# Top-32 threshold on folded scores in an attention + ELU-MLP + routed-experts kernel

## The chip, the cores and the metric

One Trainium2 chip, one core of it. The metric is the device time of one launch in microseconds (us), the median of several runs. Slots, tiles and lines are named as in the kernel; lines are those of the kernel before unless "after" is written.

## What is computed

The reference chains three stages; only the parts that matter here are shown. The change is in the mask of the attention and in the ELU.

```python
# attention: q, k, v are (4, 8, 576, 64), fp32
scores = scale * np.matmul(q, k.transpose(0, 1, 3, 2))
kth = np.partition(scores, -32, axis=-1)[..., -32:-31]   # 32nd largest of a row of 576
scores = np.where(scores >= kth, scores, -1e9)
attn = np.exp(scores - scores.max(-1, keepdims=True))
attn = attn / (attn.sum(-1, keepdims=True) + 1e-9)
x = np.matmul(attn, v)                                   # -> 2304 rows of 512
# dense MLP with ELU, 512 -> 2048 -> 512
h = x @ w_in
g = np.where(h > 0, h, np.exp(np.minimum(h, 0)) - 1)
x = g @ w_out
# then: each row is routed to the best of 8 experts (512 -> 1024 -> 512, ReLU) and weighted
```

## The kernel before, in words

Every engine has its program written out by hand (direct instructions, one queue for each engine, semaphores between them). The attention is cut into 144 **tiles**: 4 batches x 4 pairs of heads x 9 tiles (`PT_`). Tiles 0 to 7 of a pair are 128 query rows of one head, so two tiles (the two heads) make a **group** that shares its transposed result; tile 8 is mixed, with the last 64 rows of both heads. All engines walk the same list of **slots** s = 0, 1, ... (`END` of them). In slot s the engines work on different tiles, a software pipeline:

- TensorE (PE): the scores of the next group, 128x288 halves (`score`, L470) into two PSUM banks `sc`; `turn` (L489) transposes the five 128x128 pieces of `probs` of tile s-2 and, in the last tile of a group, a sixth piece with the reciprocals of the row sums (`rec_b`, L498); `weigh` (L501) multiplies a finished group by the values.
- ScalarE (ACT): `score_evac` (L673) copies the score halves to `scores` (five buffers); `expo` (L684) makes exp(scale*score - max) into `probs` (two buffers); `turned` (L691) copies the transposed tile.
- VectorE (DVE): `slot` (L890). The 32nd largest score of a row is found by MAX8 (the eight largest, L844) and MATCH_REPLACE8 (takes these eight out, L848): four MAX8 and three MATCH_REPLACE8 over all 576 scores. Tiles s and s-1 are interleaved, so that an instruction mostly waits for the one before the last. `mask` (L856) then multiplies the exponentials by (score >= 32nd largest) and sums the row; `total`, `reciprocal` and `normalise` finish a group.
- GpSimd (POOL): `widen` (L351) spreads the reciprocals; `split_x` (L344) and `split_w_in` (L360, eight times in slots 4, 8 to 32) split operands of the MLP into two parts.
- SyncE loads; it gates nothing here.

The MLP of batch b runs **beside** the attention of batch b+1: from slot `LAG` + 36 on, each slot also takes two of 71 positions of a schedule (`mlp_schedule`, L222): 16 "hidden" chunks (12 matmuls of 128x288 each), then "down" parts (3 or 4 matmuls in fp32), this twice, with the "rows" steps (transpose, sums, logits) in between and at the end. In each slot position 0 comes ahead of `turn`, position 1 behind it. A hidden chunk is turned into ELU by two ScalarE Relu (of -h and of h; the second frees the PSUM bank), an Exp, and on GpSimd `elu` (L389, two operations: e-1, then added to relu(h)). The MLP of the last batch runs after the last slot, alone (PE starts it at 910.26 us), with VectorE doing the last step of the ELU (L933). After it come the routing and the experts, which the change does not touch.

So what sets the order around the change is the place of each call in the slot loops of the four engines, and the waits. The lines of the order that count:

```python
# ScalarE, before (L759)                 # VectorE, before (slot, L890)
prep; score_evac(G, 0)  (even t)         eight(new,0); total; eight(old,2); reciprocal
x_high; mlp position 0                   bias(new); without(new,0); without(old,2)
turned(s-2)                              eight(new,1); eight(old,3); without(new,1)
score_evac(G, 1)  (odd t)                normalise; mask(old)      # new = s, old = s-1
expo(s); mlp position 1
```

Of the kernel before, what the change touches and what calls it, by code (L numbers as in the profile page):

```python
# [5 lines left out]
ALU = mybir.AluOpType  # L6
# [7 lines left out]
P = 128  # L14
TOP_K = 32
NEG = -3.0e38


def attention_moe_program(nc, q, k, v, w_in, w_out, emb, tau, w1, w2, out):
# [26 lines left out]
    LAG = 6  # L46
# [5 lines left out]
    with ctx:  # L52
# [13 lines left out]
        top = sbuf(ctx, "top", [P, 2, TOP_K])  # L66
# [21 lines left out]
        q_t = sbuf(first, "q_t", [P, 2, FULL * P])  # L88
# [4 lines left out]
        work = sbuf(first, "work", [P, 2, S])  # L93
# [4 lines left out]
        elu_e = sbuf(first, "elu_e", [P, HS])  # L98
# [33 lines left out]
        def bank(name):  # L132
# [15 lines left out]
        rowmax, exp_done, mask_done, rec_done = (  # L148
            sem("rowmax"), sem("exp_done"), sem("mask_done"), sem("rec_done"))
# [5 lines left out]
        elu_neg, elu_exp, elu_less = sem("elu_neg"), sem("elu_exp"), sem("elu_less")  # L155
# [53 lines left out]

        def x_at(t, b, pair, tok, n, parts=slice(0, P)):  # L210
            at = (NPAIR * b + pair) % RING * S + tok
            return t[parts, at:at + n]
# [3 lines left out]
        XT = 3  # L216
# [5 lines left out]
        def mlp_schedule():  # L222
# [13 lines left out]
            used, numbered = [0, 0], []  # L236
            for ops in positions:
                numbered.append([])
                for kind, blk, i, part, parts in ops:
                    bank_ = 0 if kind == "rows" else i % 2  # L240
                    if kind == "rows":

                        numbered[-1].append((kind, blk, i, used[1], 0, used[0]))
                        used[0] += 1
                        continue
                    numbered[-1].append((kind, blk, i, part, parts, used[bank_]))
                    if part == parts - 1:
                        used[bank_] += 1
            return numbered, used

        MLP_POSITIONS, BANK_USES = mlp_schedule()
# [8 lines left out]
        EARLY_SUMS = [op[5] + 1 for ops in MLP_POSITIONS for op in ops if op[0] == "rows"][RB - 1]  # L260
# [13 lines left out]
        def _(sp):  # L274
# [30 lines left out]
            sp.dma_start(work[0:E, 0, 0:DM], emb).then_inc(emb_in, 16)  # L305
# [36 lines left out]
        def _(pool):  # L342
# [7 lines left out]

            def widen(G):  # L351
# [37 lines left out]
            def elu(mb, m, pos):  # L389
                for kind, blk, i, *_ in mlp_at(m, pos):  # L390
                    if kind == "hidden":
                        chunk = FC * 2 * mb + (FC * blk + i)
                        e, r = elu_e[:, :], g[:, i * HS:(i + 1) * HS]
# [705 lines left out]
```

## Time and profile before

| | |
|---|---|
| median of 3 runs | 1387.83 us (1387.81 to 1389.81) |
| the profiled execution's own time | 1388.3 us |
| its span in the profile (first to last instruction) | 1386.6 us |
| busy, share of the span: PE, DVE, ACT, POOL | 88%, 67%, 39%, 18% |
| mean granted TensorE clock | 0.931 of full speed |

How to read it: the profile is one execution, so its instructions add up to the span of 1386.6 us; what lies around the span is 1.7 us. The busy shares are averages over stages that are limited by different engines, so the table of stretches and the timeline of one engine say more than they do. The "busy" time of an instruction goes from its start to its result; on all engines the next instruction may start before that, so costs are read from the distance of two starts. Of a group "idle before" is time in which its engine did nothing ahead of it.

### The profile page before, as it was taken

How to read it: one execution, taken by the hardware profiler on the slowest of the kernel's cores; microseconds unless marked ns; L12 is line 12 of the kernel's file. 1: busy time of each engine (PE TensorE's matmuls, PEld its weight loads, DVE VectorE, ACT ScalarE, POOL GpSimd, SP SyncE). 2: the span in 40 equal slices, each digit the busy share in tenths (PEclk: the TensorE clock that was granted, in tenths of full speed). 3: DMA queues.
4: the chain of work that ended last, by engine and by line, in shares of the span. 5: the costliest groups of instructions: out<-in, count | busy, mean ns of one | idle time of the engine just before them, and what ended most of it. 6: DMA issues, size and time to landing. Idle time of an engine off the chain costs nothing.

```text
span 1386.6 us, 21604 instructions
## 1 busy us (share of the span) xinstructions
PE 1213.3 (88%) x7809; PEld 937.1 (68%) x7810; DVE 932.9 (67%) x2320; ACT 543.0 (39%) x1243; POOL 247.0 (18%) x391
## 2 busy tenths in 40 slices
PE   3656666799999999999999999999984999999996
PEld 2444444586787786687777677797864777677773
DVE  4999999999999999999999999610226110011100
ACT  3433443574474565465466456251620000000000
POOL 0212111140151042033023024000000111111111
PEclk9866666799999999999999999999996999999998
DMA  3141100100100100001011000000160354415100
GB/s 112 37 142 48 26 17 10 27 10 18 32 21 18 44 10 18 23 22 27 9 36 26 10 13 7 1 18 0 48 230 16 119 188 157 150 64 214 69 32 21
DMA packets 80121, 72.48 MB, mean 52 GB/s; under 512 B 60310, under 2 KB 60310, under 8 KB 79520
## 3 DMA queue, kind: packets, MB, share of 16 engines
q1 hardware_dynamic: 73584, 56.13, 12.9%
q0 software_dynamic: 3760, 10.49, 2.3%
q10 hardware_dynamic: 2688, 4.72, 1.2%
q8 instruction: 50, 0.82, 0.2%
q14 instruction: 39, 0.32, 0.1%
HBM read 61.88 MB, written 11.27 MB: 53 GB/s over the span
## 4 chain that ended last, share of the span: by engine, by line
PE 52%; DVE 36%; issue 5%; ACT 3%; POOL 2%; DMA 0%; SPq 0%; DVEq 0%; ACTq 0%; POOLq 0%
DVE work L848 15%; DVE top L844 14%; PE mlp L543 12%; PE sc L643 11%; PE pv_ps L653 10%; PE mlp L534 8%; DVE probs L859 5%; PE pv_ps L515 3%; PE sc L486 3%; PE tp L494 1%; POOL g L398 1%; PE mlp L552 1%; PE tp L623 1%; PE prep_ps L559 1%; POOL elu_e L396 1%
## 5 line engine op out<-in xcount | busy, mean ns | idle before, releaser
L844 DVE MAX8 top<-work 128x8 f32<-128x576 f32 x432 | 310.1, 744 | 0.1
L543 PE MATMUL mlp<-g,wout 128*128 128x288 f32 x1024 | 270.0, 411 | 0.0
L543 PEld LDWEIGHTS mlp<-g,wout 128*128 128x128 f32 x1024 | 187.7, 190 | 61.9 <-issue 17.4
L848 DVE MATCH_REPLACE8 work<-top,work 128x576 f32<-128x576 f32 x288 | 213.0, 740 | 0.0
L698 ACT COPY probs_t<-tp 128x640 f32<-128x640 f32 (+1 forms) x144 | 108.3, 752 | 191.2 <-PE tp L498 151.7
L494 PE MATMUL tp<-ident,probs 128*128 128x128 f32 x720 | 117.5, 300 | 59.0 <-DVE probs L859 59.0
L534 PE MATMUL mlp<-x_h,win_h 128*128 128x288 f32 x512 | 162.5, 317 | 0.1
L643 PEld LDWEIGHTS sc<-xg_t,w_exp 128*128 128x128 f32 x1344 | 154.6, 193 | 11.3 <-issue 11.3
L643 PE MATMUL sc<-xg_t,w_exp 128*128 x1344 | 154.9, 276 | 1.3 <-ACT act_tick L807 1.3
L534 PE MATMUL mlp<-x_h,win_l 128*128 128x288 f32 x512 | 151.5, 296 | 0.0
L534 PE MATMUL mlp<-x_l,win_h 128*128 128x288 f32 x512 | 151.5, 296 | 0.0
L494 PEld LDWEIGHTS tp<-ident,probs 128*128 128x128 f32 x720 | 93.7, 154 | 84.1 <-DVE probs L859 69.0
L682 ACT COPY scores<-sc 128x288 f32<-128x288 f32 x288 | 103.7, 407 | 114.6 <-PE sc L486 68.2
L653 PE MATMUL pv_ps<-w_exp,h_t 128*128 128x512 f32 x336 | 147.7, 592 | 0.0
L515 PE MATMUL pv_ps<-probs_t,vals 128*64 128x128 f32 (+1 forms) x1600 | 119.3, 307 | 15.4 <-DVE x_f L884 11.6
L515 PEld LDWEIGHTS pv_ps<-probs_t,vals 128*64 128x64 f32 x1600 | 99.3, 162 | 47.5 <-issue 34.5
L859 DVE SCALAR_TENSOR_TENSOR probs<-scores,top,probs 128x576 f32<-128x576 f32 x144 | 123.9, 861 | 0.5
L844 DVE MAX8 top<-scores 128x8 f32<-128x576 f32 x144 | 108.5, 754 | 20.6 <-ACT scores L682 20.3
L486 PE MATMUL sc<-k_t,q_t 64*128 64x288 f32 x512 | 114.7, 517 | 3.9 <-ACT scores L682 3.1
L688 ACT ACTIVATE probs<-scores,negmax 128x576 f32<-128x576 f32 x144 | 114.1, 792 | 0.0
L1067 DVE TENSOR_SCALAR y_all<-pv_ps,slots 128x512 f32 x21 | 15.8, 751 | 142.2 <-PE pv_ps L653 142.2
L653 PEld LDWEIGHTS pv_ps<-w_exp,h_t 128*128 128x128 f32 x336 | 62.2, 190 | 70.3 <-issue 70.3
(159 smaller groups left out, 1400.5 us busy)
## 6 DMA issues: line engine op xcount, KB each, us to landing
w_exp<-in_moe_w SPq DMA_DIRECT2D x16, 2048.0 KB, 13.7
x_rows<-g ACTq DMA_DIRECT2D x24, 192.0 KB, 2.1
raw_qk<-in_q SPq DMA_DIRECT2D x32, 128.0 KB, 2.4
raw_qk<-in_k SPq DMA_DIRECT2D x32, 128.0 KB, 2.4
vals<-in_v SPq DMA_DIRECT2D x32, 128.0 KB, 2.3
g<-in_moe_w_in SPq DMA_DIRECT2D x4, 1024.0 KB, 5.3
wout<-in_moe_w_out SPq DMA_DIRECT2D x1, 4096.0 KB, 15.9
raw_qk<-in_q SPq DMA_DIRECT2D x32, 16.0 KB, 2.2
```

What stands on the lines that cost most here:

```text
L486: pe.matmul(sc[n % 2][:, 0:HS], q_t[of, p % 2, g_ * P:(g_ + 1) * P], k_t[of, p % 2, keys], start=True, stop=True).then_inc(sc_half, 1)
L494: last = pe.transpose(tp[:, c * P:(c + 1) * P], probs[:, T % 2, c * P:(c + 1) * P], ident[:, :])
L515: mm = pe.matmul(pv_ps[of, 0:n], vals[:, p % 2, c, of], probs_t[:, buf, at:at + n], start=(c == 0), stop=(c == NCH - 1))
L534: mm = pe.matmul(mlp_ps[bank_][:, 0:HS], wp[:, c, i * P:(i + 1) * P], x_at(xp, mb, c, blk * HS, HS), start=(k_ == 1), stop=(k_ == 3 * KD))
L543: mm = pe.matmul(mlp_ps[bank_][:, 0:HS], wout[:, c, i * P:(i + 1) * P], g[:, c * HS:(c + 1) * HS], start=(c == 0), stop=(c == FC - 1))
L643: mm = pe.matmul(sc[half][:, fi * P:(fi + 1) * P], w_exp[:, par, c * F + f * P:c * F + (f + 1) * P], xg_t[:, bass.ds((s % 2) * (KD * P) + ...
L653: mm = pe.matmul(pv_ps[:, 0:DM], h_t[:, f, :], w_exp[:, par, KD * F + f * DM:KD * F + (f + 1) * DM], start=(f == 0), stop=(f == EC - 1))
L688: act.activation(probs[:, T % 2, 0:S], scores[:, T % NSC, :], ACT.Exp, bias=negmax[:, T % 2:T % 2 + 1], scale=SCALE).then_inc(exp_done, 1)
L698: act.copy(probs_t[:, T % 3, 0:n], tp[:, 0:n]).then_inc(pt_evac, 1)
L844: chain.mark(dve.max(top[:, T % 2, 8 * r:8 * r + 8], src))
L848: chain.mark(dve.match_replace(out=w_, in_to_replace=top[:, T % 2, 8 * r:8 * r + 8], in_values=scores[:, T % NSC, :] if r == 0 else w_, im ...
L859: dve.scalar_tensor_tensor(out=pr, in0=scores[:, T % NSC, :], scalar=top[:, T % 2, TOP_K - 1:TOP_K], in1=pr, op0=ALU.is_ge, op1=ALU.mult, ...
```

## The change

- **Fold.** A row of 576 is cut into two halves of 288, and each pair of scores is ordered: VectorE writes `larger_of` = max of the pair (`larger`, one input from `scores`, the other straight from the PSUM bank `sc`), GpSimd writes `smaller_of` as a + b - larger on the bits as 32-bit integers (`both_halves`, `smaller`). The 32nd largest of the row comes from the 32 largest of `larger_of` (four MAX8, three MATCH_REPLACE8 over 288) and the 16 largest of `smaller_of` (two MAX8, one MATCH_REPLACE8 over 288): `meet` takes the minimum of each pair of ranks, `threshold` the maximum of these 17.
- **Mask.** Ahead of the exponential: ScalarE writes relu(2^100 * (threshold - score)) into `probs` (`drop`), GpSimd subtracts it from the scores (`mask`), and ScalarE's `expo` makes the exponential in place and sums the row.
- `total` (+1e-9) moves from VectorE to GpSimd.
- **ELU.** One ScalarE Relu (of -h) instead of two, an Exp, and one VectorE operation max(e - 1, h) with h from PSUM; GpSimd's two operations go. The PSUM bank of a hidden chunk is now freed by that VectorE operation (`g_done`).
- **Pipeline.** `turn`, `turned`, `total`, `widen` one slot later (s-3), `drop`, `mask`, `expo` for tile s-2; scores are made two slots ahead, both halves in one slot; `LAG` 6 to 7, `XT` 3 to 4; `q_t` has one buffer, and the third `prep` step comes at the end of a pair's slot 6, just ahead of the next pair's first scores.

```diff
-    LAG = 6
+    LAG = 7
-        q_t = sbuf(first, "q_t", [P, 2, FULL * P])
+        q_t = sbuf(first, "q_t", [P, FULL * P])
-        work = sbuf(first, "work", [P, 2, S])
+        larger_of = sbuf(first, "larger_of", [P, 4, HS])
+        smaller_of = sbuf(first, "smaller_of", [P, 3, HS])
@@ gpsimd
+            def both_halves(T):
+                wait(pool, sc_evac, scores_of(T))
+                wait(pool, thr_done, T - 2)
+                s_ = scores[:, T % NSC, :].bitcast(I32)
+                pool.tensor_tensor(smaller_of[:, T % 3, :].bitcast(I32), s_[:, 0:HS], s_[:, HS:S], ALU.add).then_inc(summed_up, 1)
+            def smaller(T):
+                wait(pool, summed_up, T + 1)
+                wait(pool, larger_done, T + 1)
+                m_ = smaller_of[:, T % 3, :].bitcast(I32)
+                pool.tensor_tensor(m_, m_, larger_of[:, T % 4, :].bitcast(I32), ALU.subtract).then_inc(folded, 1)
-                        pool.tensor_scalar(e, e, -1.0, 1.0, ALU.add, ALU.mult).then_inc(elu_less, 1)
-                        pool.tensor_tensor(r, r, e, ALU.add).then_inc(g_done, 1)
+            def mask(T):
+                pr = probs[:, T % 2, 0:S]
+                wait(pool, dropped, T + 1)
+                pool.tensor_tensor(pr, scores[:, T % NSC, :], pr, ALU.subtract).then_inc(mask_done, 1)
             for s in range(END):
-                if 0 <= s - 2 < NT and ends_group(s - 2):
-                    widen(group_of(s - 2))
+                if 0 <= s - 3 < NT and ends_group(s - 3):
+                    total(group_of(s - 3))
+                if 0 <= s - 2 < NT:
+                    mask(s - 2)
+                if s + 1 < NT:
+                    both_halves(s + 1)
+                if 0 <= s - 3 < NT and ends_group(s - 3):
+                    widen(group_of(s - 3))
+                if s + 1 < NT:
+                    smaller(s + 1)
@@ tensor, in score: a bank is free when it has been folded, not only copied
+                    wait(pe, larger_done, PT_ * p + 2 * g_ - 1 + hh if hf == 0 else 0)
@@ tensor, slot loop
-                if 3 <= t < 6 and p + 1 < NP:
-                    prep(p + 1, t - 3)
-                if starts_group(s) and G < NP * GP:
+                if t in (5, 6) and p + 1 < NP:
+                    prep(p + 1, t - 5)
+                G = scored_in(s)
+                if G is not None:
                     score(G, 0)
                 if step := mlp_slot(s):
                     mlp(*step, 0)
-                back = s - 2
+                if G is not None:
+                    score(G, 1)
+                back = s - 3
                 if 0 <= back < NT:
                     turn(back)
-                if ends_group(s) and G < NP * GP:
-                    score(G, 1)
@@ scalar
+            def drop(T):
+                wait(act, thr_done, T + 1)
+                wait(act, tr_done, T - 1)
+                act.activation(probs[:, T % 2, 0:S], scores[:, T % NSC, :], ACT.Relu,
+                               bias=thr[:, T % 2, 1:2], scale=-BIG).then_inc(dropped, 1)
             def expo(T):
-                wait(act, rowmax, T + 1)
-                act.activation(probs[:, T % 2, 0:S], scores[:, T % NSC, :], ACT.Exp,
-                               bias=negmax[:, T % 2:T % 2 + 1], scale=SCALE).then_inc(exp_done, 1)
+                wait(act, mask_done, T + 1)
+                wait(act, rec_done, G - 1)
+                act.activation(probs[:, T % 2, 0:S], probs[:, T % 2, 0:S], ACT.Exp,
+                               bias=negmax[:, T % 2:T % 2 + 1], scale=SCALE,
+                               accum_out=rowsum[:, G % 2, head_of(T):head_of(T) + 1]).then_inc(exp_done, 1)
-                        act.activation(e, mlp_ps[bank_][:, 0:HS], ACT.Relu, scale=-1.0).then_inc(elu_neg, 1)
-                        act.activation(g[:, i * HS:(i + 1) * HS], mlp_ps[bank_][:, 0:HS],
-                                       ACT.Relu).then_inc(mlp_free[bank_], 1)
+                        act.activation(at, mlp_ps[bank_][:, 0:HS], ACT.Relu, scale=-1.0).then_inc(elu_neg, 1)
@@ vector
+            def larger(T):
+                n = score_at(group_of(T), 1, head_of(T))
+                wait(dve, sc_evac, n + 1)
+                dve.tensor_tensor(larger_of[:, T % 4, :], scores[:, T % NSC, 0:HS], sc[n % 2][:, 0:HS],
+                                  ALU.max).then_inc(larger_done, 1)
+            def meet(T):
+                pairs = top[:, T % 2, 15:49].rearrange("p (k t) -> p t k", k=2)
+                chain.mark(dve.tensor_reduce(top[:, T % 2, 49:66], pairs, AX_X, ALU.min), ("meet", T))
-                        dve.scalar_tensor_tensor(out=r, in0=e, scalar=-1.0, in1=r,
-                                                 op0=ALU.add, op1=ALU.add).then_inc(g_done, 1)
+                        dve.scalar_tensor_tensor(out=at, in0=at, scalar=-1.0, in1=mlp_ps[i % 2][:, 0:HS],
+                                                 op0=ALU.add, op1=ALU.max).then_inc(g_done, 1)
```

In the lists below a row is a line, an operation, its tiles (output<-inputs) and shape, and in brackets the semaphores that it waits for. **VectorE, one slot that has no matmul chunk beside it.** Before:

```order
L844 MAX top<-scores 128x8 [waits sc_evac]
L844 MAX top<-work 128x8 [waits dve_step]
L853 TENSOR_SCALAR negmax<-top 128x1 [waits dve_step]
L848 MATCH_REPLACE work<-top,scores 128x576
L848 MATCH_REPLACE work<-top,work 128x576 [waits dve_step]
L844 MAX top<-work 128x8 [waits dve_step] x2
L848 MATCH_REPLACE work<-top,work 128x576 [waits dve_step]
L859 SCALAR_TENSOR_TENSOR probs,rowsum<-scores,top,probs 128x576 [waits exp_done,dve_step]
```

and with the change (lines of the kernel after):

```order
L918 MAX top<-larger_of 128x8 [waits larger_done]
L923 MATCH_REPLACE larger_of<-top,larger_of 128x288 [waits dve_step]
L914 TENSOR_TENSOR larger_of<-scores,sc 128x288 [waits sc_evac]
L918 MAX top<-larger_of 128x8 [waits dve_step]
L923 MATCH_REPLACE larger_of<-top,larger_of 128x288 [waits dve_step,folded]
L923 MATCH_REPLACE larger_of<-top,larger_of 128x288 [waits dve_step]
L918 MAX top<-smaller_of 128x8
L918 MAX top<-larger_of 128x8 [waits dve_step] x2
L937 TENSOR_REDUCE top<-top 128x17 [waits dve_step]
L930 TENSOR_SCALAR negmax<-top 128x1 [waits exp_done,dve_step]
L923 MATCH_REPLACE smaller_of<-top,smaller_of 128x288 [waits dve_step]
L943 TENSOR_REDUCE thr<-top 128x1 [waits dropped,dve_step]
```

Seven operations over 576 scores have become ten over 288, one fold and small ones; the pass with two SBUF operands (L859) is gone, and a wait for GpSimd (`folded`) stands in the slot. **ScalarE, a slot with two hidden chunks and scores to copy** (from the place of `turned` of the slot before). Before:

```order
L728 ACTIVATE elu_e<-mlp 128x288 [waits mlp_done1,g_done]
L729 ACTIVATE g<-mlp 128x288
L732 ACTIVATE elu_e<-elu_e 128x288 [waits elu_neg]
L682 COPY scores<-sc 128x288 [waits sc_half,mask_done] x2
L728 ACTIVATE elu_e<-mlp 128x288 [waits mlp_done0,g_done]
L729 ACTIVATE g<-mlp 128x288
L732 ACTIVATE elu_e<-elu_e 128x288 [waits elu_neg]
L698 COPY probs_t<-tp 128x768 [waits pv_done,tr_done]
L688 ACTIVATE probs<-scores,negmax 128x576 [waits tr_done,rowmax]
```

With the change:

```order
L731 ACTIVATE probs<-scores,thr 128x576 [waits tr_done,thr_done]
L724 COPY scores<-sc 128x288 [waits sc_half,mask_done] x2
L777 ACTIVATE g<-mlp 128x288 [waits mlp_done0]
L779 ACTIVATE g<-g 128x288 [waits elu_neg]
L724 COPY scores<-sc 128x288 [waits sc_half] x2
L750 COPY probs_t<-tp 128x768 [waits pv_done,xn_done,tr_done]
L739 ACTIVATE probs,rowsum<-probs,negmax 128x576 [waits rec_done,mask_done]
L777 ACTIVATE g<-mlp 128x288 [waits mlp_done1]
L779 ACTIVATE g<-g 128x288 [waits elu_neg]
```

The mask term (L731) comes first in the slot, the four score copies follow in the same slot, two of them behind a wait for `mask_done`, which GpSimd now gives and not VectorE. **GpSimd, a slot that ends a group and the next one**, with the change; before, GpSimd had one row (L355, `rec_b`) for a group and two for each hidden chunk:

```order
L367 TENSOR_SCALAR rowsum<-rowsum 128x2 [waits exp_done]
L426 TENSOR_TENSOR probs<-scores,probs 128x576 [waits dropped]
L384 TENSOR_TENSOR smaller_of<-scores 128x288 [waits thr_done,sc_evac]
L373 COPY rec_b<-rowrec 128x128 [waits rec_done]
L391 TENSOR_TENSOR smaller_of<-smaller_of,larger_of 128x288 [waits larger_done,summed_up]
```

The copy of the reciprocals, which TensorE's sixth transpose waits for, now stands behind two GpSimd operations of the newer tiles.

## Rows read from the trace of the kernel before

**Rows 1.** The page: its span, and busy tenths in 40 equal slices (PE, VectorE).
```profile
span 1386.6 us, 21604 instructions
PE   3656666799999999999999999999984999999996
DVE  4999999999999999999999999610226110011100
```

**Rows 2.** Busy time by stretch: us, PE, PEld, DVE, ACT, POOL busy, PEclk, DMA share, GB/s.
```profile
21.20:265.80 244.60, 157.35 (x881) 105.33 (x881) 244.19 (x610) 99.85 (x197) 38.87 (x42) 0.71 0.16 45
282.40:500.80 218.40, 207.02 (x1490) 163.72 (x1490) 213.08 (x534) 124.39 (x295) 52.02 (x88) 0.99 0.09 23
500.80:720.60 219.80, 209.55 (x1498) 165.84 (x1497) 214.12 (x533) 125.30 (x297) 52.75 (x88) 0.98 0.09 23
```

**Rows 3.** Timeline of VectorE, 161 to 165.5 us: start us, us, engine, line, op.
```profile
161.02 0.73 DVE L844 MAX8 top<-work 128x8 f32<-128x576 f32 x1
161.68 0.13 DVE L853 TENSOR_SCALAR negmax<-top 128x1 f32<-128x1 f32 x1
161.73 0.07 DVE L848 MATCH_VALUE_LOAD work<-top,scores 128x8 f32 x1
161.80 0.73 DVE L848 MATCH_REPLACE8 work<-top,scores 128x576 f32<-128x576 f32 x1
162.46 0.07 DVE L848 MATCH_VALUE_LOAD work<-top,work 128x8 f32 x1
...
165.23 0.28 DVE L884 TENSOR_TENSOR x_f<-pv_ps,probs_t 128x128 f32<-128x128 f32 x1
165.43 0.80 DVE L859 SCALAR_TENSOR_TENSOR probs<-scores,top,probs 128x576 f32<-128x576 f32 x1
```

**Rows 4.** Single lines, VectorE: duration ns min/median/max, first and last start.
```profile
L859 DVE SCALAR_TENSOR_TENSOR probs<-scores,top,probs x144: 796/808/2327, 29.3 to 886.1; 128x576 f32<-128x576 f32 x144
L869 DVE TENSOR_SCALAR rowsum<-rowsum x80: 122/149/730, 36.3 to 887.0; 128x2 f32<-128x2 f32 x64, 128x1 f32<-128x1 f32 x16
L853 DVE TENSOR_SCALAR negmax<-top x144: 121/131/153, 21.9 to 879.0; 128x1 f32<-128x1 f32 x144
```

**Rows 5.** Groups by line and form: busy us, mean ns, idle before and its releaser.
```profile
L688 ACT ACTIVATE probs<-scores,negmax 128x576 f32<-128x576 f32 x144 | 114.1, 792 | 0.0
L398 POOL TENSOR_TENSOR g<-g,elu_e 128x288 f32<-128x288 f32 x96 | 82.1, 855 | 8.0
L396 POOL TENSOR_SCALAR elu_e<-elu_e 128x288 f32<-128x288 f32 x96 | 44.5, 464 | 189.1 <-ACT elu_e L732 189.1
L348 POOL TENSOR_TENSOR x_l<-x_f,x_h 128x576 fp32r<-128x576 f32 x16 | 22.5, 1409 | 11.9 <-ACT x_h L708 11.9
```

**Rows 6.** Timeline of ScalarE in a slot with hidden chunks.
```profile
600.39 0.45 ACT L732 ACTIVATE elu_e<-elu_e 128x288 f32<-128x288 f32 x1
600.72 0.81 ACT L698 COPY probs_t<-tp 128x768 f32<-128x768 f32 x1
601.40 0.42 ACT L682 COPY scores<-sc 128x288 f32<-128x288 f32 x1
```

**Rows 7.** Timeline of PE: weigh, scores, one hidden chunk (first matmul), transposes, scores.
```profile
602.38 1.31 PE L515 MATMUL pv_ps<-probs_t,vals 128*64 128x128 f32 x20
603.63 0.76 PE L486 MATMUL sc<-k_t,q_t 64*128 64x288 f32 x4
604.31 0.40 PE L534 MATMUL mlp<-x_h,win_h 128*128 128x288 f32 x1
...
606.02 0.71 PE L494 MATMUL tp<-ident,probs 128*128 128x128 f32 x5
606.65 0.76 PE L486 MATMUL sc<-k_t,q_t 64*128 64x288 f32 x4
```

**Rows 8.** Timelines of VectorE and PE: masks that end slots 41 and 143, and the tail's start.
```profile
265.03 0.81 DVE L859 SCALAR_TENSOR_TENSOR probs<-scores,top,probs 128x576 f32<-128x576 f32 x1
882.78 0.80 DVE L859 SCALAR_TENSOR_TENSOR probs<-scores,top,probs 128x576 f32<-128x576 f32 x1
895.50 6.82 PE L543 MATMUL mlp<-g,wout 128*128 128x288 f32 x27
910.26 0.61 PE L534 MATMUL mlp<-x_h,win_h 128*128 128x288 f32 x1
```

More of the change, by code:

```diff
@@ L856, in mask, with folds @@
-            def mask(T):
-                pr, G = probs[:, T % 2, 0:S], group_of(T)
-                wait(dve, exp_done, T + 1)
-                dve.scalar_tensor_tensor(out=pr, in0=scores[:, T % NSC, :], scalar=top[:, T % 2, TOP_K - 1:TOP_K],
-                                         in1=pr, op0=ALU.is_ge, op1=ALU.mult,
-                                         accum_out=rowsum[:, G % 2, head_of(T):head_of(T) + 1]).then_inc(mask_done, 1)
+            def folds(T, half):
+                return smaller_of[:, T % 3, :] if half else larger_of[:, T % 4, :]
@@ new lines, in without @@
+            def without(T, half, r):
+                w_ = folds(T, half)
+                chain.until(("eight", T, half, r))
+                chain.mark(dve.match_replace(out=w_, in_to_replace=ranks(T, half, 8 * r, 8 * r + 8), in_values=w_,
+                                             imm_value=NEG), ("without", T, half, r))
+            def bias(T):
+                chain.until(("eight", T, 0, 0))
+                wait(dve, exp_done, T - 1)
+                chain.mark(dve.tensor_scalar(negmax[:, T % 2:T % 2 + 1], top[:, T % 2, 0:1], -SCALE, None, ALU.mult),
+                           ("bias", T))
@@ new lines, in meet, with threshold @@
+            def meet(T):
+                chain.until(("eight", T, 0, 3))
+                pairs = top[:, T % 2, 15:49].rearrange("p (k t) -> p t k", k=2)
+                chain.mark(dve.tensor_reduce(top[:, T % 2, 49:66], pairs, AX_X, ALU.min), ("meet", T))
+            def threshold(T):
+                chain.until(("meet", T))
+                chain.until(("bias", T))
+                wait(dve, dropped, T - 1)
+                chain.mark(dve.tensor_reduce(thr[:, T % 2, 0:1], top[:, T % 2, 49:66], AX_X, ALU.max),
+                           ("threshold", T))
@@ L898, in slot @@
-                if summed is not None:
-                    total(summed)
+                    wait(dve, larger_done, new + 1)
+                    eight(new, 0, 0)
                 if old is not None:
-                    chain.settled(1 if new is not None else 0)
-                    eight(old, 2)
+                    without(old, 0, 1)
+                if s + 1 < NT and starts_group(s + 1):
+                    larger(s + 1)
                 if summed is not None:
                     reciprocal(summed)
+                if old is not None:
+                    chain.until(("without", old, 0, 1))
+                    eight(old, 0, 2)
@@ L905, in slot @@
                 if new is not None:
-                    chain.settled(1 if old is not None else 0)
-                    bias(new)
-                    without(new, 0)
+                    wait(dve, folded, new + 1)
+                    without(new, 0, 0)
                 if old is not None:
-                    chain.settled(1 if new is not None else 0)
-                    without(old, 2)
+                    without(old, 0, 2)
+                if s + 1 < NT and starts_group(s + 1) and not mixed(s + 1):
+                    larger(s + 2)
@@ L920, in slot @@
-                    without(new, 1)
+                    chain.until(("without", new, 0, 0))
+                    eight(new, 0, 1)
+                if old is not None:
+                    meet(old)
+                    bias(old)
+                if new is not None:
+                    without(new, 1, 0)
+                if old is not None:
+                    threshold(old)
+                if new is not None:
+                    chain.until(("without", new, 1, 0))
+                    eight(new, 1, 1)
```

187 lines of the change are left out of this document (99 added, 88 removed).

## The prediction

> **What bounds the kernel now.** I read the page first. VectorE is at 9 tenths in slices 2 to 25 of 40 and mostly idle after; PE climbs to 9 in slice 9 and stays near it [rows 1]. So there are three parts: slots without MLP work, slots with it, and a tail that belongs to PE. The table of stretches gives their limits [rows 2]. In the first part VectorE is busy 244.19 of 244.60 us, PE 157.35 at a granted clock of 0.71: VectorE alone sets the pace. In the second, 36 slots take 218.40 and 219.80 us; VectorE is busy 213 to 214 of them and PE 207 to 210, at a clock of 0.98 to 0.99. **Two engines are full there**, so a faster VectorE can win at most what PE leaves idle, some 10 us for each 36 slots, less what PE's records overstate (they are modelled, and each reaches past the next start). The stages are cut by the masks that end slots 41 and 143: 21.20 to 265.8 (42 slots, 5.82 each) and to 883.6 (102 slots, 617.8 us, 6.06 each) [rows 2, 8].
>
> **Part 1: VectorE's work for a tile.** Costs are distances of starts [rows 3]. MAX8 over 576: 161.68 - 161.02 = 0.66. MATCH_REPLACE8: 162.46 - 161.80 = 0.66, plus 0.07 for its load. A 128x1 operation: 0.05. The 128x128 operation with a PSUM operand: 0.20, that is 0.133 for 128 elements at one each 1.04 ns (600 ns for 576 fits MAX8 likewise) and 0.065 fixed. Before: 4 x 0.66 + 3 x 0.73 + mask 0.81 + small ones about 0.2 = 5.85, which is the slot. A row of 288 is 0.30 shorter. No row shows a MAX8 over 288; it costs between 0.36 (only the elements count) and 0.44 (its whole duration, 0.73 - 0.30, with no overlap). I take 0.364, since two starts in a row here are 0.66 apart at a duration of 0.73. After: 6 MAX8 x 0.364 = 2.18; 4 MATCH_REPLACE8 x 0.43 = 1.70; fold 0.37; meet, threshold, bias, scale 0.05 to 0.10 each = 0.29; reciprocal and normalise 0.15; two places where an instruction follows the one it needs, 0.04. Sum **4.72**. The ELU step on VectorE adds 0.37 a chunk, so a slot with two hidden chunks costs 5.46.
>
> The port: the mask pass with two SBUF operands took up to 2.33 us beside a long GpSimd operation, mean 0.861 (123.9 us in 144) at a median of 0.808 [rows 4]. That is gone, worth 0.05 a slot, and is in the 5.82 and 6.06 above.
>
> **Part 2: GpSimd.** It goes from 18% busy to the mask 1.41, two operations over 288 and 0.27 of small ones. The float form with two inputs takes 0.80 to 0.86, the one with a scalar 0.43 to 0.46 [rows 5]; for the integer form there is no row, so I bound it by 0.43 and 1.6 (twice the float) and take 0.80, the nearest in operands and shape. Sum 3.3 a slot, below 4.72: cover for it exists, but its results are waited for.
>
> **Part 3: ScalarE.** Adds the mask term, 0.79 busy and about 0.68 between starts, as the copies of this kind [rows 5, 6], saves one Relu a chunk (0.3 between starts, as the copy of 288). Its mean load goes from 3.4 to about 3.9 a slot: not a limit, but it works in order, and two copies of scores now stand behind `mask_done`.
>
> **Slots without MLP (43 now, LAG is 7).** VectorE 4.72. The chain beside it for two slots: mask term 0.7, GpSimd mask 1.4, copy of the second score half-pair, PE's score (at the lower clock about 1.3 for a pair), transposes about 1.3 and the sixth, copy 0.7, exponential 0.8, next mask term, mask, exponential: about 9.4 to 9.9 for two slots against 9.44. I take 4.85 a slot. The eight `split_w_in` steps (3.4 us of GpSimd each) now delay `folded`: about 0.6 us each, 5 in all. The start has a fold ahead, 2. So 43 x 4.85 + 5 + 2 = 215.6 against 244.6: **-29.0**.
>
> **Slots with MLP (101 now).** PE's own work: chunk 1.71, one score half-pair 0.68, five transposes 0.63, weigh 1.25 [rows 7]; a pair of slots with four chunks is 4 x 1.71 + 2 x 0.68 + 0.63 + 0.75 + 1.25 = 10.8, VectorE's 10.9. Then the loop that I think decides: PE ends the second chunk of a slot (0); ScalarE Relu 0.45 and Exp 0.33 to the next start [rows 6], 0.83 with the hand-over; mask term 0.75 to 1.6; GpSimd mask 1.4 to 3.1; the waiting score copy 0.35 to 3.5; second score and five transposes to 4.5; and the reciprocals arrive about then too (mask, `both_halves` 0.8, `widen` 0.3). PE's own work over that stretch is 0.68 + 1.71 + 0.68 + 0.55 = 3.6. So PE waits **0.9 us in every pair of hidden slots**; there are 8 pairs in 36 slots: 7 us. In the down parts the ScalarE work ahead of the mask term is missing, and the loop comes out at 10.2 for two slots, as PE's own 10.2 to 11.8: no wait. At the end of each pair of heads PE waits for the third `prep` copy, about 0.8, four times: 3. PE's need itself I take as 205 of the 208 busy. 205 + 7 + 3 = 215 for 36 slots, 5.97 each: 101 x 5.97 = 603.0 against 617.8: **-14.8**.
>
> **Edges.** The MLP starts one slot later, so one step more is left for the end: 8 fp32 matmuls = 16 records at 6.82 / 27 = 0.25: **+4.0** [rows 8]. In the tail a chunk's bank is now freed by VectorE: Relu 0.45, Exp 0.45, VectorE 0.5 and hand-overs, about 1.5 against the 1.6 of the next chunk: covered barely, **+1** for 32 chunks. Routing and experts: nothing changes. SyncE's loads have fewer waits in front: nothing.
>
> Sum: -29.0 - 14.8 + 4.0 + 1.0 = -38.8. The span goes from 1386.6 to 1347.8; the profiled execution's time is 1.7 above its span and 0.5 above the median, so **1349**.
>
> **A rule against the change.** Two starts are 0.66 apart at a duration of 0.73 [rows 3]. The Trainium skill ("VectorE: DVE Perf Modes", The DRAIN you can't avoid) says instead that after each VectorE operation the next one does not start until the pipe is empty. The row speaks against it for 576 scores, where 0.07 overlaps. Were the overlap lost at 288, each operation would cost its whole duration; that is rival C.
>
> **Rivals.**
> A. *No waits in the loop.* ScalarE and GpSimd run ahead of PE, and PE is simply full: 5.75 a slot, 4.75 in the first part. 1349 - 101 x 0.22 - 43 x 0.10 = 1322; with the split steps hidden, 1317. For it: PE's chain has slack from slot to slot in the trace. Against: the list of ScalarE puts the mask term behind the second chunk's Exp. Chance 0.15.
> B. *The loop is longer*, because ScalarE's waits (score copy behind `mask_done`, then the chunk, then the transposed tile) also hold VectorE's ELU step, and so the bank: 6.25 a slot, 1349 + 101 x 0.28 = 1377. Chance 0.13.
> C. *Slower: short VectorE operations pay their full duration.* Place: all ten MAX8 and MATCH_REPLACE8 and the small ones, some 15 a slot. At 0.08 each a slot costs 5.9 and with two chunks 6.8: 43 x 1.2 = 52 in the first part; in the second, above slacks of about 0.4 in hidden slots and 0.45 in half of the others, 45 x 1.0 + 28 x 0.75 = 66. 1349 + 115 about 1465. It decides from 0.04 an operation on, where it eats the whole gain of 39. Chance 0.07.
> D. *The integer operations are slow on GpSimd*, 1.6 each: each 0.1 on one lengthens the two-slot loop by 0.1, so 0.4 x 43 + 0.29 x 101 = 46: 1395, slower by 0.5%. Chance 0.07.
> E. *The port again.* VectorE's two 128x1 operations a tile could wait for GpSimd, which is now busy 60% of the time: about 0.3 each, 26 in the first part and 15 in the second, 1390. The 128x2 form took up to 0.730, but the 128x1 form never over 0.153 in 144 [rows 4]. The Trainium skill ("SBUF — State Buffer", Who interferes with whom) calls the shared pair an exclusive lock; the 2.33 us [rows 4] agree. Chance 0.05.
>
> The rest, 0.53, is the forecast: 1335 to 1362. The change does what it says: there is no VectorE pass with two SBUF operands left in a tile, so I give no chance to that.
>
> **Chances and range.** Within 0.2% (2.8 us), about what a measurement can tell, lies the edge between B and D: 0.04. Faster: 0.53 + 0.15 + most of B = 0.77. Slower: C, D, E = 0.19. The range takes in A and reaches past D and E: 1315 to 1398; outside are C and the ends of the others.
>
> **What would show it.** Right: VectorE's MAX8 starts 0.36 apart in the first part and slots of 4.7 to 4.9 there; PE waiting about 0.9 every second hidden slot for scores (`scores` copies) or for `rec_b`; 36 slots in 213 to 217 us. Wrong: MAX8 starts 0.44 apart (C); `smaller_of` operations near 1.6 (D); 128x1 operations of 0.5 (E); PE never waiting (A); VectorE idle ahead of the ELU step (B).

## Result: 6.3% slower, where 2.9% faster was forecast

| | before | with the change |
|---|---|---|
| median | 1388.82 us (1387.81 to 1390.28, 4 runs) | 1476.74 us (1469.54 to 1484.83, 4 runs) |
| ratio, 95% interval | | 1.0634 [1.0577, 1.069] |
| span of the profiled execution | 1386.6 us | 1475.2 us |

The forecast was 1349 us, with a range to 1398. The page of the changed kernel (compare [rows 1]; the fourth line is the granted clock of TensorE in tenths):

```profile
span 1475.2 us, 23823 instructions
PE   4665665679989989899988998999995899999996
DVE  4776866778978668887776887811034211000000
PEclk9756656689999989999998999999997899999998
```

VectorE, at 9 in 24 slices before, is at 9 in one. So the work did leave it, and the time was not won. The stretches (columns as in [rows 2]: busy PE, PEld, DVE, ACT, POOL, clock) are the 43 slots without MLP, and twice 36 slots with it:

```profile
23.80:298.50 274.70, 175.11 (x860) 114.56 (x861) 204.25 (x851) 129.66 (x274) 163.71 (x190) 0.64 0.13 37
328.90:564.10 235.20, 213.38 (x1498) 167.25 (x1497) 187.11 (x762) 148.91 (x336) 119.83 (x153) 0.97 0.09 21
564.10:802.30 238.20, 216.32 (x1499) 170.11 (x1499) 187.32 (x762) 148.87 (x336) 119.93 (x153) 0.96 0.09 21
```

36 slots take 235 to 238 us where they took 218 to 220, and the first part 275 for 43 slots where it took 245 for 42. No engine fills the first part now: VectorE, the busiest, works 204 of 275 us. In the 36 slots PE still works 213 of 235. What the operations themselves cost is as it was priced. VectorE's timeline (start, us, operation):

```profile
149.91 0.44 DVE L918 MAX8 top<-larger_of 128x8 f32<-128x288 f32 x1
150.27 0.07 DVE L923 MATCH_VALUE_LOAD larger_of<-top,larger_of 128x8 f32 x1
150.33 0.44 DVE L923 MATCH_REPLACE8 larger_of<-top,larger_of 128x288 f32<-128x288 f32 x1
150.69 0.08 DVE L923 MATCH_VALUE_LOAD larger_of<-top,larger_of 128x8 f32 x1
```

A MAX8 over 288 starts 0.36 before the next instruction and lasts 0.44. The groups by line (busy, mean ns, idle before and its releaser) and two single lines (ns min/median/max):

```profile
L384 POOL TENSOR_TENSOR smaller_of<-scores 128x288 int32<-128x288 int32 x144 | 114.5, 795 | 18.9 <-ACT scores L724 18.9
L426 POOL TENSOR_TENSOR probs<-scores,probs 128x576 f32<-128x576 f32 x144 | 203.1, 1410 | 327.7 <-ACT probs L731 322.3 <-DVE thr L948 4.8
L724 ACT COPY scores<-sc 128x288 f32<-128x288 f32 x288 | 107.0, 398 | 140.9 <-PE sc L523 90.4 <-POOL probs L426 40.9 <-PE sc L515 9.2
L955 DVE RECIPROCAL rowrec<-rowsum 128x2 f32<-128x2 f32 (+1 forms) x80 | 13.2, 165 | 130.7 <-POOL rowsum L367 130.7
L535 PE MATMUL tp<-ident,rec_b 128*128 128x128 f32 x80 | 27.5, 343 | 75.3 <-POOL rec_b L373 75.3
```
```profile
L930 DVE TENSOR_SCALAR negmax<-top x144: 138/145/155, 28.8 to 960.9; 128x1 f32<-128x1 f32 x144
L948 DVE TENSOR_SCALAR thr<-thr x144: 133/135/153, 29.8 to 961.4; 128x1 f32<-128x1 f32 x144
```

The integer operation takes 0.795 us, GpSimd's mask 1.41, and no 128x1 operation was held up, with GpSimd busy 38% of the span. The idle columns tell where the time went: PE stands 75.3 us ahead of the sixth transpose, the one of the reciprocals (before, this idle time came to 36.8 us, beside a VectorE that was full or nearly so); VectorE stands 130.7 us for the row sum of GpSimd; ScalarE 40.9 us for GpSimd's mask, ahead of score copies.

**One boundary between two pairs of heads**, from the timelines of PE, ScalarE and GpSimd:

```profile
176.54 0.79 POOL L384 TENSOR_TENSOR smaller_of<-scores 128x288 int32<-128x288 int32 x1
177.28 0.29 POOL L373 COPY rec_b<-rowrec 128x128 f32<-128x128 f32 x1
177.62 0.33 PE L535 MATMUL tp<-ident,rec_b 128*128 128x128 f32 x1 [2.85 <-POOL rec_b L373]
178.84 2.40 PE L552 MATMUL pv_ps<-probs_t,vals 128*64 128x128 f32 x20 [0.89 <-ACT probs_t L750]
181.17 0.69 PE L500 MATMUL prep_ps<-ident,raw_qk 128*128 128x128 f32 x2
181.90 0.21 ACT L711 COPY q_diag<-prep_ps 64x64 f32<-64x64 f32 x1 [2.34 <-PE prep_ps L500]
182.44 0.78 ACT L731 ACTIVATE probs<-scores,thr 128x576 f32<-128x576 f32 x1
```

The reciprocals (L373) wait behind `smaller_of`, PE waits for them (2.85), then weighs, and only then makes the third q/k step; ScalarE, in order, waits for that (2.34) and comes to the mask term last, though its threshold had been there for 3.9 us. The distance from one tile's threshold (L948, at 183.02) to the next (193.38) is 10.4 us here, against 4.3 to 5.6 in a plain slot. Such long ones (8 to 12 us) come two to four times in each pair of the first part.

### The profile page after: what moved, and what is told of

It reads as the page before. It is cut to its first block, busy times and chain, and to the rows that moved or that the text cites. A ratio compares the mean times of both kernels' runs of the same rounds, so it can differ in the third digit from the quotient of the medians.

```text
span 1475.2 us, 23823 instructions
## 1 busy us (share of the span) xinstructions
PE 1257.7 (85%) x7809; PEld 962.2 (65%) x7810; DVE 815.9 (55%) x3201; ACT 635.5 (43%) x1403; POOL 555.7 (38%) x711
## 3 DMA queue, kind: packets, MB, share of 16 engines
q1 hardware_dynamic: 73584, 56.13, 12.1%
q10 hardware_dynamic: 2688, 4.72, 1.1%
## 4 chain that ended last, share of the span: by engine, by line
PE 58%; issue 19%; POOL 12%; ACT 7%; DVE 2%; DMA 0%; SPq 0%; POOLq 0%; DVEq 0%; ACTq 0%
PE mlp L581 12%; PE sc L683 10%; PE pv_ps L693 10%; PE mlp L572 9%; PE pv_ps L552 5%; PE sc L523 5%; POOL smaller_of L384 4%; ACT probs L739 3%; POOL smaller_of L391 2%; PE tp L531 2%; PE tp L535 1%; POOL x_l L360 1%; ACT probs_t L750 1%; ACT scores L724 1%; POOL rec_b L373 1%
## 5 line engine op out<-in xcount | busy, mean ns | idle before, releaser
L426 POOL TENSOR_TENSOR probs<-scores,probs 128x576 f32<-128x576 f32 x144 | 203.1, 1410 | 327.7 <-ACT probs L731 322.3
L918 DVE MAX8 top<-larger_of 128x8 f32<-128x288 f32 x576 | 245.8, 448 | 0.9
L923 DVE MATCH_REPLACE8 larger_of<-top,larger_of 128x288 f32<-128x288 f32 x432 | 189.3, 444 | 0.0
L523 PE MATMUL sc<-k_t,q_t 64*128 64x288 f32 x512 | 140.0, 547 | 39.8 <-ACT scores L724 25.7
L572 PE MATMUL mlp<-x_l,win_h 128*128 128x288 f32 x512 | 155.4, 303 | 0.0
L531 PE MATMUL tp<-ident,probs 128*128 128x128 f32 x720 | 126.3, 315 | 20.8 <-ACT probs L739 20.8
L1029 DVE SCALAR_TENSOR_TENSOR g<-g,mlp 128x288 f32<-128x288 f32 x128 | 57.8, 452 | 146.4 <-ACT g L779 146.1
L918 DVE MAX8 top<-smaller_of 128x8 f32<-128x288 f32 x288 | 131.8, 458 | 0.0
L384 POOL TENSOR_TENSOR smaller_of<-scores 128x288 int32<-128x288 int32 x144 | 114.5, 795 | 18.9 <-ACT scores L724 18.9
L523 PEld LDWEIGHTS sc<-k_t,q_t 64*128 64x128 f32 x512 | 58.3, 222 | 94.2 <-ACT scores L724 57.2
```

Source lines behind the costliest of these rows:

```text
L384: pool.tensor_tensor(smaller_of[:, T % 3, :].bitcast(I32), s_[:, 0:HS], s_[:, HS:S], ALU.add).then_inc(summed_up, 1)
L426: pool.tensor_tensor(pr, scores[:, T % NSC, :], pr, ALU.subtract).then_inc(mask_done, 1)
L523: pe.matmul(sc[n % 2][:, 0:HS], q_t[of, g_ * P:(g_ + 1) * P], k_t[of, p % 2, keys], start=True, stop=True).then_inc(sc_half, 1)
L531: last = pe.transpose(tp[:, c * P:(c + 1) * P], probs[:, T % 2, c * P:(c + 1) * P], ident[:, :])
L572: mm = pe.matmul(mlp_ps[bank_][:, 0:HS], wp[:, c, i * P:(i + 1) * P], x_at(xp, mb, c, blk * HS, HS), start=(k_ == 1), stop=(k_ == 3 * KD))
L918: chain.mark(dve.max(ranks(T, half, 8 * r, 8 * r + 8), folds(T, half)), ("eight", T, half, r))
```

## Experiments

Theory **R**: the loop exponential, row sum, reciprocal, `widen`, sixth transpose, copy, exponential sets the pace, because `widen` stands behind the mask and `both_halves` of newer tiles. Theory **P**: the boundary of a pair does, because q/k steps stand ahead of the mask term. Beside the times I read from each trace four points: the threshold of tile 41 (end of the part without MLP; in the kernel before, the MLP begins one slot earlier), the 36 slots from tile 43 to 79, the start of the tail on PE, and the tail. The profile is one execution of each kernel, and the granted clock of TensorE was not the same in all of them (last section).

| run | median us | to tile 41 | tiles 43 to 79 | tail starts | tail |
|---|---|---|---|---|---|
| before (mask in place of threshold) | 1388.8 | 270.9 | 218.3 | 910.3 | 476.3 |
| the change | 1476.7 | 298.0 | 236.7 | 992.9 | 482.3 |
| e1_term_first | 1465.7 | 283.1 | 238.5 | 977.9 | 485.0 |
| e2_prep_early | 1439.0 | 281.4 | 227.5 | 952.5 | 485.0 |
| e3_widen_first | 1403.6 | 281.4 | 222.1 | 919.9 | 481.8 |
| e4_short_mask | 1450.8 | 259.9 | 222.1 | 904.1 | 541.0 |
| e5_both | 1370.9 | 261.1 | 211.6 | 882.8 | 481.7 |
| e6_widen_last | 1530.6 | 310.0 | 252.0 | 1048.4 | 482.3 |
| e7_exp_first | 1375.6 | 259.5 | 214.8 | 890.8 | 484.7 |
| e9_quarters | 1375.5 | 254.7 | 218.3 | 891.3 | 482.3 |
| e10_recip_later | 1381.5 | 260.8 | 218.4 | 897.7 | 482.0 |
| e11_quarters_recip | 1377.6 | 257.0 | 218.4 | 894.1 | 482.0 |
| e12_both_short_mask | 1411.7 | 244.1 | 213.7 | 870.7 | 540.2 |

**The order at the boundary.** ScalarE's slot loop:

```diff
-                if t in (5, 6) and p + 1 < NP:
-                    prep(p + 1, t - 5)
                 if 0 <= s - 2 < NT:
                     drop(s - 2)
+                if t in (5, 6) and p + 1 < NP:
+                    prep(p + 1, t - 5)
```

> ScalarE takes the mask term of tile s-2 ahead of the q/k copies in slots 5 and 6 of a pair of heads, nothing else. Theory P (the boundary of a pair): in the trace of the changed kernel two of the three long intervals of a pair (8.9 and 10.2 us against 4.3 to 5.6) begin with the mask term stuck behind a copy that waits for PE; this one order should give back about 3 us at slot 5 and 1 at slot 6 in 15 pairs: 1477 to about 1430, and the interval of 8.9 us at slot 6 falls to under 6. Theory R (VectorE waits for the row sums in every second slot): within 10 us of 1477, the waits move elsewhere.

Measured: 1465.68 us (1453.3 to 1467.28), 1.0531 [1.048, 1.0582] of the kernel before: 11 us less than the change, a quarter of what P asked. In addition, PE and ScalarE take the third step early:

```diff
                 if G is not None:
                     score(G, 1)            # score_evac(G, 1) on ScalarE
+                if t == 6 and p + 1 < NP:
+                    prep(p + 1, 2)
                 back = s - 3
...
-                if t == 6 and p + 1 < NP:
-                    prep(p + 1, 2)
```

> As the one before, and the third q/k step (PE and ScalarE) moved from the end of slot 6 to ahead of the transposes there. Theory P: the interval of 10.2 us at slots 7 and 8 also falls to about 6, another 3 to 4 us in 15 pairs, about 1380 to 1400 in all. Theory R: not under 1455.

Measured: 1438.98 us (1437.09 to 1439.46), 1.0358 [1.0341, 1.0375]. Together the two orders give 38 us, 2.5 us for each of 15 boundaries. The boundary is real, and about half as dear as P had it; R's bounds, within 10 us of 1477 for e1 and not under 1455 for e2, do not hold either. So the change pays in two places, and the second one is this.

**The place of `widen`.** GpSimd's slot loop:

```diff
                 if 0 <= s - 3 < NT and ends_group(s - 3):
                     total(group_of(s - 3))
+                    widen(group_of(s - 3))
                 if 0 <= s - 2 < NT:
                     mask(s - 2)
                 if s + 1 < NT:
                     both_halves(s + 1)
-                if 0 <= s - 3 < NT and ends_group(s - 3):
-                    widen(group_of(s - 3))
                 if s + 1 < NT:
                     smaller(s + 1)
```

> GpSimd spreads the reciprocals directly behind the row sums, ahead of the mask and of both_halves, nothing else. Theory R: PE's idle time ahead of the sixth transpose (162.8 us summed over PE and its weight loads, some 80 of PE) falls by two thirds and the time by 40 to 60 us, to about 1425. Theory P: PE's wait there is what follows from the late mask term, and the time falls by less than 15 us.

Measured: 1403.56 us (1403.28 to 1403.92), 1.0107 [1.0091, 1.0124]. **One line moved gives back 73 of the 88 us.** The other way round, `widen` behind `smaller`:

> As the change, but the reciprocals are spread behind smaller, one more GpSimd operation of 0.8 us (and a hand-over) late. Theory R: the loop through the sixth transpose sets the pace in nearly every one of 80 groups, so the time grows by 55 to 75 us, to about 1540. Rival: it is critical only in hidden slots and at boundaries, some 35 groups: 1500 at most.

Measured: 1530.55 us (1523.98 to 1534.17), 1.1002 [1.0968, 1.1037], 54 us more. PE's sixth transpose, by form, in e6_widen_last, in e3_widen_first and in e5_both (each from its own list of groups):

```profile
L535 PE MATMUL tp<-ident,rec_b 128*128 128x128 f32 x80 | 29.0, 362 | 117.6 <-POOL rec_b L373 117.6
```
```profile
L534 PE MATMUL tp<-ident,rec_b 128*128 128x128 f32 x80 | 24.6, 308 | 7.4 <-POOL rec_b L373 7.4
```
```profile
L534 PE MATMUL tp<-ident,rec_b 128*128 128x128 f32 x80 | 24.0, 300 | 1.9 <-POOL rec_b L373 1.8
```

PE's wait goes 117.6, 75.3, 7.4 us as `widen` moves forward. How many of the 80 groups wait is in the views of that line, for e6_widen_last, the change and e3_widen_first:

```profile
  POOL rec_b L373: 117.6, 48
```
```profile
  POOL rec_b L373: 75.3, 46
```
```profile
  POOL rec_b L373: 7.4, 5
```

So in the change PE stands there in 46 of 80 groups, 1.6 us each, mostly three of the five groups of a pair: 13 of 22 up to tile 41, 11 of 20 in each 36 slots. One GpSimd operation of 0.8 us later costs 54 us, and 42 of these are longer waits in this place. Theory R holds in its kind: the place of `widen` decides, in the part without MLP too (tile 41 comes 16.6 us sooner with e3, 12.0 later with e6). In size it was off: it asked 40 to 60 us of e3 and "nearly every one of 80 groups" of e6; the waits are fewer and longer than that. A part of the 73 us is the clock's: in the 36 slots of tiles 43 to 79, where both kernels were granted 0.96 of full speed, e3 gains 14.6 us; in tiles 79 to 115, with 1.00 for 0.96, it gains 22.3.

**Both.** e1, e2 and e3 together:

> The mask term ahead of the q/k copies, the third q/k step ahead of the transposes, and the reciprocals spread directly behind the row sums: the two orders that gave 38 and 73 us alone. If boundary and reciprocal are two separate waits, they add up: 1477 - 111 = about 1366, faster than the kernel before. If the boundary's stall was partly the same time as PE's wait for the reciprocals, about 1375 to 1385.

Measured: **1370.93 us (1366.2 to 1377.19), 0.988 [0.9841, 0.9919] of the kernel before**: 1.2% under it. 38 + 73 = 111 would be the sum, 106 were found: the two waits are separate in the main. The four runs lie at 1366 (twice), 1375 and 1377, the first two at the sum and the others where the overlap of the two was expected, so a small overlap is not excluded.

**The kernel before with the late q/k steps alone** (slots 5 and 6, the third at the end of 6, nothing else):

```diff
-                if 3 <= t < 6 and p + 1 < NP:
-                    prep(p + 1, t - 3)
+                if t in (5, 6) and p + 1 < NP:
+                    prep(p + 1, t - 5)
...
+                if at_t == 6 and pair + 1 < NP:
+                    prep(pair + 1, 2)
```

> The kernel before with only the q/k steps moved as in the change: slots 5 and 6, the third at the end of slot 6 (two buffers of q kept). If the late place itself costs, it is 2 us or more a pair of heads and 1389 becomes 1420 or more; if it costs only together with scores made two slots ahead and a term that stands behind it, within 8 us of 1389.

Measured: 1389.72 us (1386.29 to 1391.24), 0.9998 [0.9988, 1.0007]. The place by itself costs nothing there. It costs in the change, where the first scores of the next pair are made at once behind it and a mask term stands behind it in ScalarE's order; that these two make the difference is argued from the timeline above. The kernel before also has two buffers of q, and a VectorE that is busy 244.19 of 244.60 us in the first part [rows 2], beside which the other engines have slack; no run separates these.

**How much of it is GpSimd's mask.**

```diff
-                pr = probs[:, T % 2, 0:S]
+                pr = probs[:, T % 2, 0:P]
...
-                pool.tensor_tensor(pr, scores[:, T % NSC, :], pr, ALU.subtract).then_inc(mask_done, 1)
+                pool.tensor_tensor(pr, scores[:, T % NSC, 0:P], pr, ALU.subtract).then_inc(mask_done, 1)
...
-                               bias=thr[:, T % 2, 1:2], scale=-BIG).then_inc(dropped, 1)
+                               bias=negmax[:, T % 2:T % 2 + 1], scale=1.0).then_inc(dropped, 1)
```

> GpSimd's mask operation takes 128 columns in place of 576 (about 0.45 us for 1.41), and the term is the Relu of the scores, so nothing is masked; all waits stay. Theory M (the loop runs through GpSimd's mask in every slot): about 0.5 to 0.9 us in each of 144 slots, 1477 to 1350 to 1405. Theory P: the mask lies on the chain only where the boundary has used up the slack, 15 pairs times 2 to 3 masks, 1430 to 1450.

> e5_both with GpSimd's mask over 128 columns in place of 576 and the Relu of the scores as the term (nothing is masked, all waits stay): what GpSimd's 1.41 us still costs once the two orders are mended. The forecast wanted 1349; e5_both has 1371, and its first part 5.6 us a slot against the 4.85 of the forecast. Theory G: the rest is the chain term, mask, exponential, row sum, reciprocal, and the copies behind the mask: the first part falls to 4.9 a slot (30 us) and the MLP part by under 10, 1371 to about 1335. Rival: the rest is PE at its lower clock and the q/k copies: 1360 or more.

Measured: 1450.82 us (1447.06 to 1459.29), 1.0468 [1.043, 1.0507], and 1411.65 us (1408.14 to 1412.82), 1.0147 [1.0128, 1.0166]; the second is *slower* than e5_both, from which it takes work away. The totals can't be used: without the mask other numbers reach the router, and the experts' loop runs over more tiles. The matmuls of the experts, in the change and in e12_both_short_mask:

```profile
L683 PE MATMUL sc<-xg_t,w_exp 128*128 x1344 | 156.2, 278 | 1.4 <-ACT act_tick L858 1.4
```
```profile
L682 PE MATMUL sc<-xg_t,w_exp 128*128 x1600 | 184.6, 277 | 2.3 <-ACT act_tick L857 1.4 <-DMA w_exp<-in_moe_w 1.0
```

1344 / 64 = 21 tiles against 25, and a tail of 540 against 482 us. So the two are compared at the start of the tail. From the change the short mask takes 992.9 - 904.1 = 88.8 us, 0.62 a slot (theory M's 0.5 to 0.9): GpSimd's mask lies on the way of the slots too. From e5_both it takes 12.1: 17 us in the first part, and nothing in tiles 43 to 79 (211.6 to 213.7), though there the granted clock was 0.98 against 1.00, so the two do not compare cleanly. Theory G wanted 30 in the first part. **What an operation on the way costs depends on the order around it, and not on its length alone.**

**What is left in e5_both.** Three tries, and two of them together, none better:

```diff
 # e7: ScalarE, exponential of s-2 ahead of the copy of s-3
-                if 0 <= back < NT:
-                    turned(back)
                 if 0 <= s - 2 < NT:
                     expo(s - 2)
+                if 0 <= back < NT:
+                    turned(back)
 # e9: GpSimd, w_in split in 16 steps
-                if 4 <= s < 4 + 4 * 2 * KD and s % 4 == 0:
-                    split_w_in(*divmod((s - 4) // 4, 2))
+                if 4 <= s < 4 + 2 * 4 * KD and s % 2 == 0:
+                    split_w_in(*divmod((s - 4) // 2, 4))
 # e10: VectorE, reciprocal later
-                if summed is not None:
-                    reciprocal(summed)
                 if old is not None:
                     chain.until(("without", old, 0, 1))
                     eight(old, 0, 2)
+                if summed is not None:
+                    reciprocal(summed)
```

> As e5_both, and ScalarE makes the exponential of tile s-2 ahead of the copy of the transposed tile s-3. Theory R carried on (the row sum, which the exponential gives, is what VectorE waits for, 107 us in widen_first): the sum comes one copy (0.7 us) sooner and VectorE waits less, 10 to 30 us under e5_both. Rival: the copy that comes later holds the weighing on PE and the buffers of the transposes, and it is slower than e5_both.

> As e5_both, with the split of w_in on GpSimd in sixteen steps of 512 columns (about 1.8 us each) in slots 4, 6 to 34, in place of eight of 1024 (3.4 us) in slots 4, 8 to 32. Theory S: in the slots without MLP each long step delays the mask, and with it the score copies behind it, by more than the slack of a slot (a copy waits 3.0 us in the trace of e5_both), while half of it fits: 1371 falls by 10 to 25 us. Rival: GpSimd's total is what counts there, which stays: within 5 us.

> As e5_both, VectorE takes the reciprocal behind the third MAX8 of the older tile, 0.36 us later in its order. If VectorE's wait for the row sum sets the pace, some of it is filled with work: 3 to 10 us less. If GpSimd, PE or ScalarE sets it, the later reciprocal only delays GpSimd: 0 to 10 us more.

> e9_quarters and e10_recip_later together: the sum of the two differences from e5_both, within 4 us.

Measured: e7 1375.64 us (1373.13 to 1379.42), 0.9898 [0.9874, 0.9923]; e9 1375.53 (1365.71 to 1376.94), 0.9877 [0.9833, 0.9921]; e10 1381.49 (1380.0 to 1382.93), 0.9939 [0.9917, 0.9961]; e11 1377.55 (1367.59 to 1377.89), 0.9887 [0.9845, 0.9929]. By the medians e7 can't be told from e5_both. In its profile, at the same full clock as in e5_both's, it gains 1.6 us up to tile 41 and loses 3.2 in the 36 slots, so there the rival's description fits. e10 lies 11 us above e5_both, as its rival allowed, but the profiles don't put that down to the reciprocal: up to tile 41 the two are equal (260.8 and 261.1), and the loss begins in the MLP part, at a lower clock (0.96 of full speed in these 36 slots, 1.00 in e5_both). e11 is 9 us below the sum of the differences of e9 and e10, which it should have met within 4. Up to tile 41 the split gains 6.4 us (254.7 for 261.1), where theory S wanted 10 to 25 of the whole; the 36 slots that follow lost 6.7, without any change of their code. In all e9 is within 5 us of e5_both, as its rival said. In e5_both the price of a long split step is to be seen (GpSimd, then ScalarE):

```profile
158.78 2.35 POOL L400 TENSOR_TENSOR win_l<-g,win_h 128x1024 fp32r<-128x1024 f32 x1
161.09 1.40 POOL L426 TENSOR_TENSOR probs<-scores,probs 128x576 f32<-128x576 f32 x1
162.52 0.70 ACT L723 COPY scores<-sc 128x288 f32<-128x288 f32 x2 [3.02 <-POOL probs L426]
```

ScalarE had the mask term ready at 158.57. The mask starts 2.5 us later, behind the split, and ScalarE stands 3.02 us ahead of the score copy that waits for the mask.

## Why the prediction was wrong, point by point

- **VectorE's work: right.** 0.36 from start to start for 288, no dearer (rival C needed 0.40); plain slots of e5_both take mostly 4.3 to 5.1 us, about the 4.72 of the sum. The sentence of the Trainium skill that rival C came from ("VectorE: DVE Perf Modes", The DRAIN you can't avoid) does not fit at 288 or at 576: 0.08 of each operation lies under the next. The same section goes on to say that a next operation that is not held starts earlier, and that does fit; the prediction took only its first half. Rival D falls (0.795 us), rival E falls (0.155 at most).
- **The failed step: "the reciprocals arrive about then too (mask, `both_halves` 0.8, `widen` 0.3)"**, and its companion "in the down parts ... no wait". I saw PE wait for them, priced the wait at 0.9 us and gave it to 8 pairs of slots in 36; for the down parts and the part without MLP I took none, and let the loop take 9.4 to 9.9 us there. Measured: PE stood 15 us in each 36 slots where I had 7, in 11 of 20 groups at 1.4 us, and 32.0 us up to tile 41 where I had nothing, in 13 of 22 groups at 2.5 us. Moving that one copy ahead of `mask` and `both_halves` gives 73 us, over half of the miss of 127 us of span. I also did not carry the wait on: VectorE's reciprocal stands early in VectorE's slot and waits for GpSimd's sum (130.7 us, in 74 of 80 groups), so VectorE can't run ahead there. How much of the 73 us comes through this is not shown: with e3 this wait is still 106.9 us, and a later reciprocal (e10) moved nothing up to tile 41.
- **Mis-sized: "PE waits for the third `prep` copy, about 0.8, four times: 3"**, and nothing at all for it in the part without MLP. The two orders gave 38 us, 2.5 a boundary.
- **Mis-sized: `split_w_in` 0.6 us each.** The wait of 3.02 us above is behind one; halving the steps gave 6.4 us in that part, where all eight had been put at 5.
- **By parts of the sum.** Without MLP: forecast 215.6, measured 277 (298.2 - 21.1). With MLP: 603.0 against 660.6. Up to the tail 3.5 more than the edge said, and in the tail 6.0 in place of 1.0: a chunk now takes 1.66 and 1.72 us in turn for 1.58 to 1.60, and PE stands 1.5 us before each of three "rows" steps, for 0.80 to 0.86 before.
- **Rivals.** B named the right kind of thing (waits in the loop of in-order queues), but at 28 us, which would still have been faster, and at 0.13; the slower side was given to prices of operations (C, D, E), all wrong. C's sum comes to 1467, not 1465.
- **With the other orders: a hit in part by luck.** With `widen` and the q/k steps in other places the same work takes 1370.9, inside the forecast's range of 1315 to 1398, though 22 above its value. But the parts miss in opposite ways: in e5_both's profile the part without MLP takes 240.2 us against 215.6, and the part with it 588.7 against 603.0. So the price list of the operations held, and the estimate of what the waits leave did not, in either part.
- **What stays open.** The first part of e5_both is 24.6 us above its forecast, and the short mask shows that 17 of them hang on GpSimd's mask. More score buffers, which would take the copies off the mask, or two buffers of q, with which the q/k steps could go back to slots 3 to 5, were not tried.

## What to carry to other kernels

When work moves to an in-order engine, list for every result on the way from one slot to the next what stands *ahead of it in that queue*, and add up the whole round trip, all ways round, beside each engine's busy time. An instruction that somebody waits for goes first in its queue, ahead of longer work on newer tiles: here one 0.3 us copy behind two operations cost 73 us. A queue that can't run ahead (here VectorE, idle 130.7 us at the reciprocal) may then pass one engine's delay on to the others; this step is read from the order, and no run shows it alone.

## Not expected of the hardware

**Near-equal kernels ran at different granted clocks.** 36 slots with MLP, whose code is the same, in e5_both and in e9_quarters (columns as in [rows 2]):

```profile
272.40:484.10 211.70, 204.84 (x1500) 162.96 (x1498) 186.05 (x762) 147.81 (x337) 121.78 (x153) 1.00 0.10 24
```
```profile
265.90:484.20 218.30, 211.65 (x1498) 168.71 (x1496) 186.27 (x761) 147.82 (x337) 121.87 (x153) 0.96 0.10 23
```

At the same place of the schedule (the boundary of a pair at which PE transposes tiles 74 to 76) in e5_both, in e9_quarters and in the change:

```profile
471.00:479.00 8.00, 7.11 (x62) 5.77 (x63) 5.75 (x24) 6.08 (x16) 3.65 (x4) 1.00 0.42 100
```
```profile
466.00:475.00 9.00, 8.11 (x43) 6.23 (x44) 4.74 (x20) 4.95 (x14) 3.34 (x4) 0.50 0.37 88
```
```profile
532.00:542.00 10.00, 8.37 (x43) 6.09 (x43) 5.43 (x22) 4.67 (x13) 3.78 (x6) 0.50 0.18 46
```

The clock (third number from the end) is 1.00 in the first, the 2.4 GHz level, and 0.50, so 1.2 GHz, in the others, after a stretch in which PE was partly idle: 5.54 of 7.50 us busy, at 0.74, in e9_quarters just before. In e5_both it was 5.42 of 7.60 busy at 1.00, so almost the same idle time ends on either side. These 36 slots take 6.6 us more in e9_quarters, nearly all of it as longer busy time of PE.

The mean granted clock of each run, which is on record, goes with its time: e5_both had 0.937 and 0.935 at 1366 us and 0.928 and 0.925 at 1375 and 1377; e9_quarters 0.933 at 1366 and 0.919 to 0.924 at 1375 to 1377; e11 0.926 at 1368 and 0.916 to 0.917 at 1377 to 1378. So e5_both and e9_quarters lie on the same two levels, and the gain of the finer split is not to be seen in the whole. Why an execution falls on one level or the other stays open: a low clock may follow from the idle time as well as add to it, and only one execution of each has a profile. Differences of 10 us between these versions are not differences of their orders alone.
